# Attention, two gated feed-forward layers: another order of values, scores and transposes beside the down products

## The reference

```python
scores = scale * q @ k.T                      # 8 heads of 64, batch 4
scores = where(0 <= row - col < 64, scores, -1e9)
attn   = exp(scores - max(scores)); attn /= sum(attn) + 1e-9
x      = attn @ v                             # (4, 576, 512)

h      = maximum(x @ w_in, 0)                 # (4, 576, 1024)
gate   = sigmoid(conv3(h))                    # 3 taps along the sequence, per channel
x2     = (h * gate) @ w_out                   # (4, 576, 512)

h      = maximum(x2 @ w_in2, 0); u, v = split(h)
v_n    = (v - mean(v)) / sqrt(var(v) + 1e-6)
out    = (u * (w_spatial @ v_n + b_spatial)) @ w_out2
```

## Time and profile before

| | us |
|---|---|
| median of 3 runs | 513.01 |
| lowest and highest of them | 510.52, 514.62 |
| the profiled execution, whole | 516.8 |
| its span, first to last instruction | 514.9 |
| TensorE matmuls busy within it | 486.9 |
| VectorE, ScalarE, GpSimd busy | 267.8, 254.5, 94.8 |
| mean granted TensorE clock, share of full speed | 0.987 |

### The profile page before, as it was taken

How to read it: one execution, slowest core, us unless ns; L and a number is a source line. 1 busy time by engine, 2 the same in 40 slices (tenths; PEclk the granted TensorE clock), 3 DMA queues, 4 the chain that set the end, 5 groups by cost and what they waited for, 6 DMA issues and landing times.

```text
span 514.9 us, 9377 instructions
## 1 busy us (share of the span) xinstructions
PE 486.9 (95%) x3784; PEld 436.4 (85%) x3784; DVE 267.8 (52%) x482; ACT 254.5 (49%) x665; POOL 94.8 (18%) x159
## 2 busy tenths in 40 slices
PE   3668979999999999999999999999999999999997
PEld 2458969878888888877899979989998899989997
DVE  2539986497547946396349644834044503440040
ACT  2865865486538755486058474335213621262212
POOL 3638312241232221241003110001000100020000
PEclk9979979999999999999999999999999999999999
DMA  8961225201430312005000500001100010002002
GB/s 253 375 211 34 72 59 179 72 0 42 144 103 2 101 44 83 1 0 205 1 1 3 193 5 1 0 1 47 46 1 2 24 69 1 0 1 93 1 0 93
DMA packets 24223, 33.03 MB, mean 64 GB/s; under 512 B 1522, under 2 KB 13810, under 8 KB 24180
## 3 DMA queue, kind: packets, MB, share of 16 engines
q1 hardware_dynamic: 22324, 29.01, 17.1%
q10 hardware_dynamic: 1856, 3.42, 1.8%
HBM read 27.71 MB, written 4.72 MB: 63 GB/s over the span
## 4 chain that ended last, share of the span: by engine, by line
PE 82%; DVE 6%; DMA 4%; issue 3%; ACT 3%; POOL 1%; SPq 0%; ACTq 0%; DVEq 0%; POOLq 0%
PE dense L391 38%; PE pt_ps L391 10%; PE score L391 9%; PE pt_ps L586 6%; PE score L586 6%; DMA qk<-q_t 4%; PE x_ps L391 4%; PE x_ps L453 3%; PE pt_ps L437 3%; PE score L423 2%; DVE tmp L889 2%; DVE wr L874 1%; ACT vp L638 1%; PE score L416 1%; DVE ar L902 1%
## 5 line engine op out<-in xcount | busy, mean ns | idle before, releaser
L391 PE MATMUL dense<-xr,wr 128*128 128x512 f32 (+2 forms) x480 | 101.4, 371 | 3.3 <-POOL wr L1117 1.7
L391 PEld LDWEIGHTS dense<-xr,wr 128*128 128x128 f32 x480 | 87.8, 188 | 16.2 <-POOL wr L1117 2.0
L391 PE MATMUL dense<-ar,wr 128*128 128x512 f32 (+2 forms) x456 | 99.3, 374 | 0.3 <-DVE wr L874 0.3
L391 PEld LDWEIGHTS dense<-ar,wr 128*128 128x128 f32 x456 | 82.4, 188 | 11.5 <-DVE wr L874 0.6
L889 DVE SCALAR_TENSOR_TENSOR tmp<-tmp,taps 128x512 f32<-128x512 f32 (+2 forms) x80 | 57.7, 722 | 22.2 <-ACT tmp L679 20.7
L1111 POOL TENSOR_TENSOR vp<-vp,recip 128x1024 f32<-128x1024 f32 x18 | 34.5, 1917 | 108.3 <-DVE recip L853 108.3
L638 ACT ACTIVATE vp<-score,bias 128x128 f32<-128x128 f32 x128 | 45.0, 382 | 1.3 <-PE pt_ps L437 0.6
L1188 POOL TENSOR_TENSOR ident<-ident,minus_half 128x1 f32<-128x1 f32 (+1 forms) x20 | 11.0, 548 | 155.5 <-DVE ident L997 155.5
L671 ACT ACTIVATE tmp<-dense 128x512 f32<-128x512 f32 (+2 forms) x40 | 21.9, 549 | 34.0 <-PE dense L391 34.0
L805 ACT ACTIVATE ar<-vp 128x576 fp32r<-128x576 f32 x16 | 11.0, 687 | 50.1 <-DVE vp L1047 50.1
L391 PE MATMUL dense<-wr,xr 128*128 128x512 f32 x144 | 33.3, 389 | 0.0
(11 more groups left out here) (97 smaller groups left out, 752.2 us busy)
## 6 DMA issues: line engine op xcount, KB each, us to landing
vp<-v_rows SPq DMA_DIRECT2D x36, 256.0 KB, 4.0
out_t<-vp SPq DMA_DIRECT2D x16, 288.0 KB, 2.1
qk<-k_t SPq DMA_DIRECT2D x9, 384.0 KB, 3.8
qk<-q_t SPq DMA_DIRECT2D x9, 384.0 KB, 5.5
x2keep<-w_in ACTq DMA_DIRECT2D x2, 1024.0 KB, 11.0
qk<-w_in SPq DMA_DIRECT2D x1, 2048.0 KB, 9.6
x2keep<-w_out ACTq DMA_DIRECT2D x1, 1280.0 KB, 11.3
vp<-w_spatial_t SPq DMA_DIRECT2D x1, 1152.0 KB
```

The lines of the kernel that those rows point to most:

```text
L391: last = mm(dst, stationary(a, t), moving(c, t), start=(t == 0 and n == 0), stop=(t == of - 1 and n == 2))
```

## The change

Two edits, one on TensorE and one on VectorE, both in the cycles of the doubles 3 to 17. TensorE does the values of n ahead of the scores of n+2. VectorE makes x's low part of double n ahead of the maximum of double n+2 (and, in the cycle of double 3, ahead of `out_low(4)`). No instruction is added or taken away. The programs of ScalarE, GpSimd and SyncE are as before.

```diff
                 for n, share in zip(CYCLES[c], SHARES[c]):
+                    values(n)
                     if n + 2 < DOUBLES:
                         scores(n + 2)
-                    values(n)
                     if n + 1 < DOUBLES:
                         transposes(n + 1)
                     for i in range(done, done + share):
@@ VectorE
                     if ending:
                         keep_x2(c, 0)
+                    x_low(n)
                     if n + 2 < DOUBLES:
                         softmax_maximum(n + 2)
                     if n == RAMP:
                         out_low(4)
-                    x_low(n)
                     if n + 1 < DOUBLES:
                         copy_transposed(n + 1)
```

## The result

The changed kernel takes 518.82 us (median of 4, 517.64 to 519.58) beside 513.74 for the kernel before (4 runs). The ratio is 1.0100, 95% interval 1.0068 to 1.0133: slower by 5.1 us, between 3.5 and 6.8.

The account below looks back on a forecast made before the run. TensorE, busy 95%, was taken as the bound, with next to no slack in the loop feeding it. Terms 1.28 + 1.80 + 0.88 = 3.96 us on the 513.0 median gave 517.0, 0.8% slower, range 513.5 to 520.3.

Parts of the forecast that it names:

- Turns, 0.60 each: Cycle after an up product, tiles 1 to 3: low part delays maximum and transposes 0.60 us each, 1.80 in all.
- Cycles with 5 pieces: Tiles 1 and 2: new waits ahead of the transposes of 11 and 15, 0.38 and 0.50 us, together 0.88.
- Tile 0: Transposes of 5 win 0.63 us, but the maximum of 6 starts 1.81 late; transposes of 7 end 1.28 later.
- TensorE's transitions: Passing from values to scores and scores to transposes: bounded by 0.1 us less to 0.2 more a cycle, taken as 0.
- SyncE's queue: Loads of v, k and q wait for values and scores, which end within the same three steps; costed at nothing.
- The clock: Tile 0's 2.98 us wait: by a rule against long gaps, values there keep the clock up, worth nothing.
- The rival in which the clock falls again in the new waits: Tile 0, cycle of double 5: several waits of about 1 us drop the clock, 3 us more, 520.0; chance 0.15.
- The rival in which the slack is more than it looks: Turns after up: low part costs nearly nothing, 1.8 us and some of 0.88 go, 514.5 to 515; chance 0.17.
- The rival in which the filled gap wins: Cycle of double 4: values in the wait win up to 2.6 us, 510.4 to 512; chance 0.08.

Follow-up runs that it names:

- e4: The changed kernel with VectorE's old order (low part behind the maximum) in the first cycle of each tile only; ratio to the kernel before 1.0028.
- e3: The kernel before with the maximum of each tile's first cycle moved into the tail of the up product on VectorE; ratio 0.9942.
- e9: The kernel before, unedited, timed against itself and profiled again; ratio 1.0004, 236.28 us from double 3's cycle to the second layer.
- e10: The kernel before, unedited, one more profiled execution; 236.32 us from double 3's cycle to the second layer.
- e6: e3 with low parts 5 to 7 of w_out moved behind the maximum and scaling of double 6 on VectorE; ratio to the kernel before 0.9937.
- e8: e6 with 14, 5, 5, 8 pieces in tile 0 instead of 13, 6, 5, 8, timed; ratio to the kernel before 0.9902, median 508.35 us.
- e1: The kernel before with TensorE's edit alone (values ahead of scores), VectorE's order as before; ratio 1.0025.
- e5: e3 with values ahead of scores on TensorE, one profiled execution; 235.05 us from double 3's cycle to the second layer.

## Why the prediction was right

The forecast was 4.0 us slower and 517.0; the stretch lost 4.09 in the pair of profiles and the median is 518.8. The mechanism is as forecast: the low part in VectorE's queue delays the maximum, and through ScalarE and GpSimd the transposes. That 4.09 lies so near 4.0 is partly luck, since the 4.0 belongs to one profile of the kernel before; against the other two the loss is 4.7. By its steps:

- *Turns, 0.60 each.* Measured 0.58, 0.57 and 0.58 (from the cycle's start to the transposes of 9, 13 and 17). The step, one low part in a queue that is late already, is shown three ways: by the trace, by e4, which wins it back, and by e3, which wins in tiles 0 and 3 by moving the maximum the other way.
- *Cycles with 5 pieces.* Forecast 0.38 in tile 1 and 0.50 in tile 2, measured 0.65 (from the transposes of 9 to those of 11: 14.17 before, 14.82 after) and 0.50. The term for tile 1 was mis-sized: I took 4.46 us from a maximum to the reciprocals from tile 0. In this cycle it is 4.75 (maximum 136.01, L850 at 140.76), because the exponentials of 11 start 0.56 us after the scaling and not 0.26. The trace of before had it too, in the cycle of the earlier trace rows: the maximum at 136.49, L850 at 141.25, 4.76.
- *Tile 0.* Forecast 1.28, measured 1.21 at the transposes of 7 and 1.24 at the next `up`; transposes of 5 forecast 0.63 earlier, measured 0.65; those of 6 forecast 1.42 later, measured 1.37; the maximum of 6 forecast 1.81 late, measured 1.79. The prediction says that GpSimd and the transposes meet in tile 0 "from double 6 on"; in its trace that holds from double 7 (the end at 87.94, the transposes at 88.08), and double 6 had 0.54 us and not 0.14, so 0.40 to spare, which its sum did use (1.81 late became 1.42). That slack came from the early fall of the clock. In e9 and e10 it is gone, and tile 0 costs 1.78. The low parts of w_out, named as what stands between, were what e6 to e8 moved with profit.
- *TensorE's transitions.* Taken as 0: measured 0 (2.29 us for the three steps in both orders).
- *SyncE's queue* cost nothing: no wait of TensorE in the cycles names a DMA.
- *The clock.* That it fell anyway with values in the gap was not foreseen; it was at 0.50 from 67 to 73 us in the changed kernel, where TensorE had been idle for 1.37, 0.43 and 1.16 us with short bursts between and never for longer. So a rule about one long gap, as the prediction draws on, does not cover this case. I had written that keeping the clock up would be worth nothing: e1 bears that out, with 1.00 throughout and the tile 0 of e9 and e10. But when the clock falls does matter: e9 and e10 price the early fall at 0.6 us in the kernel before. It is a term of the base, which the prediction carried from its one profile to the median of the runs. Of the 1.8 us between 517.0 and 518.8, this explains 0.6, and 0.7 is the median of the kernel before itself, 513.7 in that comparison for the 513.0 I started from; the rest is inside the interval.

The rival in which the clock falls again in the new waits did not come: the changed kernel's row for the stretch of the wait ahead of the transposes of 6 has 1.00, as has all of the time from 73.6 to 82 us.

```profile
78.00:80.00 2.00, 0.88 (x34) 0.66 (x25) 1.75 (x2) 0.05 (x1) 1.86 (x1) 1.00 0.00 0
```

The rival in which the slack is more than it looks fell with e4. The rival in which the filled gap wins fell with e1 and e5: at most 0.54 us in tile 0 and not 2.6, nothing against e9 and e10, and nothing once the maximum is early.

## What to carry to other kernels

Where an engine that is 50% busy feeds one that is 95% busy through a loop, look for ends that meet within 0.2 us; an instruction put ahead in a queue that is late already costs its whole length, one that ends before the queue's next input comes costs nothing (e4, tile 1), and one taken out wins only down to whatever ends next. A gap on the busy engine is worth filling only if the work behind the gap doesn't come from the same late chain; here the chain had to be shortened (maximum first, bulk work after it), and that won 1%. When two profiles of one kernel differ in their start, compare them from a fixed instruction on, and profile the kernel before more than once: here 0.5 us of a gain in tile 0 was only the base.

## What the runs showed of the hardware

- The three low parts of w_out took 3.62 us right after GpSimd's normalisation had started, and 1.89 us in e8, where they start at 68.94 and GpSimd's 1.90 us from 66.63 are over:

```profile
66.63 1.90 POOL L1113 TENSOR_TENSOR vp<-vp,recip 128x1024 f32<-128x1024 f32 x1 [9.91 <-DVE recip L853]
...
68.94 1.89 DVE L874 TENSOR_TENSOR wr<-x2keep,wr 128x512 fp32r<-128x512 f32 x3
```

The difference is 1.73 us. In the kernel before the first of the three took 2.42 us, started 0.03 after GpSimd (71.05 and 71.08), and the other two 0.60 each; the single one at 66.16 took 0.68. So one instruction waited, for about the length of the normalisation. The Trainium skill, page "SBUF — State Buffer", section "Who interferes with whom", says that a VectorE instruction with two inputs in SBUF and a GpSimd instruction that reads SBUF exclude each other, the second one waiting out the first. The trace agrees. The maximum, whose one large input is in PSUM, ran beside the normalisation of e8 at its usual 1.22 us (67.60 to 68.82).
- The same wait of 2.20 us was followed by either level of the clock, 1.41 us apart in cost (e3, e6), and the kernel before showed the fall at different moments after the same wait of 2.97 or 2.98 us. In the changed kernel, with idle pieces of 1.37 us and less, it fell 0.5 to 0.8 us after the values of 4 had begun in both profiles; in e1, e4 and e5, with pieces of 1.14 us and less, it stayed up. The cost of a gap of this length is not one number.
- The exponentials of double 11 begin 0.54 to 0.56 us after their scaling in all thirteen traces, those of the other doubles from 7 to 16 that need no table load 0.26 to 0.34. The profile names no releaser beyond the scaling, or "issue"; the cause is open.
